# The output product of batch 0 by seven products of halves, with its sums on GpSimd during the mix

## What is computed

```python
def _moe2_ref(x, w_in, w_spatial, b_spatial, w_out):
    h = np.maximum(x @ w_in, 0.0)                   # (2, 768, 1024)
    u, v = h[..., :512], h[..., 512:]
    v_n = (v - mu) / np.sqrt(var + 1e-06)           # over the 512 features
    v_s = np.einsum('ts,bsd->btd', w_spatial, v_n) + b_spatial[None, :, None]   # "the mix"
    gated = u * v_s                                 # (2, 768, 512)
    return (gated @ w_out).astype(np.float32)       # "the output product", 768x512 by 512x512 per batch
```

## Time and profile before

| quantity | value |
|---|---|
| median of three runs | 352.87 us |
| the profiled execution, its own time | 352.47 us |
| its span, first to last instruction | 350.7 us |
| PE busy over the span | 98% |
| DVE busy | 80% |
| POOL busy | 38% |
| last matmul starts | 346.19 us |

### The profile page before, as it was taken

The page is one execution under the profiler, slowest core; times in us unless marked ns, Lnnn a source line. Parts: engine busy times, 40 slices in busy tenths (PEclk is TensorE's granted clock), DMA queues, the critical chain, the costliest instruction groups (busy, mean ns, idle before and its releaser), DMA issues.

```text
span 350.7 us, 7675 instructions
## 1 busy us (share of the span) xinstructions
PE 344.1 (98%) x2890; PEld 315.4 (90%) x2891; DVE 282.0 (80%) x643; ACT 205.5 (59%) x502; POOL 132.7 (38%) x195
## 2 busy tenths in 40 slices
PE   8999999999999999999999999999999999999995
PEld 4568988999989999999989999998899999998894
DVE  6995888777877498899769999956975899949953
ACT  4986767777767489796465556444655107307440
POOL 4889898444554101200034000002464670249300
PEclk9999999999999999999999999999999999999999
DMA  7962343343314023210150000004245500031205
GB/s 234 398 241 69 100 116 91 127 129 120 115 46 168 2 74 135 93 62 0 46 196 0 0 3 0 0 2 164 81 143 155 195 1 2 5 115 61 90 32 186
DMA packets 15915, 33.29 MB, mean 95 GB/s; under 512 B 1921, under 2 KB 6529, under 8 KB 15873
## 3 DMA queue, kind: packets, MB, share of 16 engines
q1 hardware_dynamic: 15440, 32.48, 27.4%
q10 hardware_dynamic: 432, 0.26, 0.3%
HBM read 29.59 MB, written 3.15 MB: 93 GB/s over the span
## 4 chain that ended last, share of the span: by engine, by line
PE 85%; DVE 5%; POOL 5%; ACT 2%; issue 1%; DMA 1%; DVEq 0%; ACTq 0%
PE bank L2236 16%; PE bank L2282 15%; PE bank L2280 15%; PE bank L2281 15%; PE bank L2319 6%; PE bank L2215 4%; PE bank L2191 4%; PE bank L2522 3%; PE bank L2440 3%; PE bank L2317 2%; POOL p_sb L897 2%; PE bank L2145 2%; DVE p_sb L1522 2%; ACT p_sb L1056 1%; PE bank L2521 1%
## 5 line engine op out<-in xcount | busy, mean ns | idle before, releaser
L2236 PE MATMUL bank<-xT,w_hi 128*128 128x384 f32 x256 | 69.6, 345 | 0.2 <-DVE xT L1544 0.2
L897 POOL TENSOR_SCALAR p_sb<-p_sb,denom 128x256 f32<-128x256 f32 (+1 forms) x96 | 48.1, 516 | 35.7 <-DVE denom L1533 35.7
L1056 ACT ACTIVATE p_sb<-p_sb,row_min 128x256 f32<-128x256 f32 (+1 forms) x96 | 46.3, 487 | 14.6 <-DVE row_min L1522 14.6
L2236 PEld LDWEIGHTS bank<-xT,w_hi 128*128 128x128 f32 x256 | 45.7, 188 | 0.7 <-DVE xT L1544 0.4
L2236 PE MATMUL bank<-xT,w_lo 128*128 128x384 f32 x128 | 44.0, 344 | 0.0
L918 POOL TENSOR_SCALAR rstd<-mean_var 128x1 f32<-128x1 f32 x12 | 4.5, 379 | 96.8 <-DVE mean_var L1686 96.8
L1563 DVE SCALAR_TENSOR_TENSOR c_sb<-h_sb,conv_sb,c_sb 128x382 f32<-128x382 f32 (+2 forms) x56 | 37.1, 663 | 2.0
L1522 DVE CUSTOM_DVE_ANT_0 p_sb<-bank,table 128x256 f32<-128x256 f32 (+1 forms) x96 | 33.0, 398 | 5.2 <-PE bank L2145 5.1
L2191 PE MATMUL bank<-ident,p_sb 128*128 128x128 f32 x176 | 29.3, 281 | 0.4 <-POOL p_sb L897 0.2
L1064 ACT COPY pt_sb<-bank 128x512 f32<-128x512 f32 (+1 forms) x44 | 23.9, 544 | 8.5 <-PE bank L2191 8.1
L2191 PEld LDWEIGHTS bank<-ident,p_sb 128*128 128x128 f32 x176 | 20.2, 140 | 7.4 <-POOL p_sb L897 4.4
(11 more groups left out here) (265 smaller groups left out, 992.3 us busy)
## 6 DMA issues: line engine op xcount, KB each, us to landing
stage<-in_weights SPq DMA_DIRECT2D x17, 512.0 KB, 3.3
v_sb<-in_v SPq DMA_DIRECT2D x8, 390.0 KB, 3.8
k_sb<-in_k SPq DMA_DIRECT2D x8, 384.0 KB, 4.2
q_sb<-in_q SPq DMA_DIRECT2D x13, 192.0 KB, 2.4
v_sb<-in_v SPq DMA_DIRECT2D x6, 260.0 KB, 4.5
f_s_raw<-in_weights SPq DMA_DIRECT2D x3, 512.0 KB, 6.0
out_dram<-out_sb SPq DMA_DIRECT2D x6, 256.0 KB, 2.0
k_sb<-in_k SPq DMA_DIRECT2D x5, 256.0 KB, 3.3
```

The source lines that it names most:

```text
L897: nc.gpsimd.tensor_scalar(probs_h, probs_h, denom[:, u % SLOTS, h:h + 1], 1.0, ALU.mult, ALU.mult).then_inc(scaled, 1)
L1056: nc.scalar.activation(p_sb[:, u % SLOTS, h, 0:n], p_sb[:, u % SLOTS, h, 0:n], ACT.Exp, bias=row_min[:, u % SLOTS, h:h + 1], scale=-1.0, a ...
L2236: last = nc.tensor.matmul(h_bank(j)[:, 0:C], w, x, start=r == 0, stop=r == F1_GROUP - 1)
```

## The change

Batch 0's output is made like batch 1's, by one function `output(b)` that runs for both. What that needs is put elsewhere:

- POOL makes the four sums S of batch 0's gated values, `sum_o_s(0)`, as soon as batch 0's gated values and the first pass pair of the second mix are there (the fourth once S1T1 is done), ahead of batch 1's product with u.
- POOL makes the four sums T of the output weights too, after the first two of the eight products with u. DVE made them before.
- The order of products is A11B11, S4B22, S2T2, S3T3, S1T1, A22T4, A12B21 in both batches; S4B22 was fifth.
- DVE makes the rests of six (not eight) blocks of batch 0's gated values, and makes them late; it makes four more rests of sums S and fifteen more additions. ACT makes twelve more copies from bank X and four more rounded sums instead of six copies of whole tiles.
- Both batches are stored in quarters of 128 x 256, 23 of them on SP's queue and one on ACT's. Before, batch 0 had six stores of 128 x 512 and batch 1 nine.

```diff
-O_PASSES = tuple((what, i) for what in ("A11B11", "S2T2", "S3T3", "S1T1", "S4B22", "A22T4", "A12B21") for i in range(OH))
+O_PASSES = tuple((what, i) for what in ("A11B11", "S4B22", "S2T2", "S3T3", "S1T1", "A22T4", "A12B21") for i in range(OH))
-O_X_BANKS, O_BANKS = (4, 5, 6), (7, 0, 1, 2, 3)
-O_SUMS = O_SPLITS = (1, 3, 2, 4)
+O_X_BANKS, O_BANKS = (0, 5, 2), (7, 1, 6, 3, 4)
+O_SUMS, O_S_SPLITS, O_T_SPLITS = (1, 3, 2, 4), (4, 2, 3, 1), (2, 3, 1, 4)
-GT_ROUNDED = tuple((0, n) for n in range(2 * KH)) + tuple((1, k) for k in (0, 1, 4, 5, 6, 7))
-GT_RESTS = GT_ROUNDED[:2 * KH] + tuple((1, k) for k in (0, 1, 5, 7, 4, 6))
+GT_ROUNDED = tuple((0, n) for n in (0, 1, 2, 3, 6, 7)) + tuple((1, k) for k in (0, 1, 4, 5, 6, 7))
+GT_RESTS = tuple((0, n) for n in (0, 1, 6, 7, 2, 3)) + tuple((1, k) for k in (0, 1, 5, 7, 4, 6))
...
 @block.sync
-            for name, k, half, n in (("21", 1, 0, 4), ("12", 0, 1, 3), ("11", 0, 0, 1), ("22", 1, 1, 2)):
-                sp.wait_ge(mix_done, passed("A22T4" if n > 2 else "S2T2", IH - 1))
+            sp.wait_ge(mix_done, passed("S1T1", IH - 1))
+            for name, k, half, n in (("12", 0, 1, 3), ("11", 0, 0, 1), ("22", 1, 1, 2), ("21", 1, 0, 4)):
...
 @block.gpsimd
+            def sum_o_s(b):
+                s1, s2, s3, s4 = (o_s_raw_sb[b][n][:] for n in range(1, 5))
+                nc.gpsimd.tensor_tensor(s1, gt_block(b, 1, 0), gt_block(b, 1, 1), ALU.add).then_inc(o_s_raw, 1)
+                pool.wait_ge(o_s_raw, o_sum_no(b, 1))
+                nc.gpsimd.tensor_tensor(s3, gt_block(b, 0, 0), gt_block(b, 1, 0), ALU.subtract).then_inc(o_s_raw, 1)
...
+                nc.gpsimd.tensor_tensor(s2, s1, gt_block(b, 0, 0), ALU.subtract).then_inc(o_s_raw, 1)
...
+                if b == 0:
+                    pool.wait_ge(mix_done, passed("S1T1", IH - 1))
+                nc.gpsimd.tensor_tensor(s4, gt_block(b, 0, 1), s2, ALU.subtract).then_inc(o_s_raw, 1)
...
 @block.scalar
+            for n in O_S_SPLITS:
+                round_o_s(0, n)
+            for k in (0, 1):
+                round_gt(2 * KH + k)
             act_flag = path_flag(act)
-            for k in (0, 1, 4):
-                round_gt(2 * KH + k)
...
+            act.wait_ge(mix_done, passed("S2T2", IH - 1))
+            for n in O_SUMS:
+                round_o_t(n)
+            act.wait_ge(left_mix, 2 * KH + len(READS))
+            copies_of_x(0)
+            for k in (4, 5, 6, 7):
                 round_gt(2 * KH + k)
...
+            for n in O_S_SPLITS:
+                round_o_s(1, n)
+            copies_of_x(1)
...
 @block.tensor
-            for j in range(NT):
-                result(j)
-            second_output()
+            for b in range(B):
+                output(b)
...
+            def output(b):
+                rests = 6 * b
+                pe.wait_ge(gt_lo_in, rests + 2)
...
+                pe.wait_ge(gt_lo_in, rests + 4)
+                pe.wait_ge(o_t_lo_in, O_T_SPLITS.index(4) + 1)
                 for i in range(OH):
-                    wait_turn("V", i)
-                    o_pass("V", i, gated_tile(1, 1), o_t(4))
-                pe.wait_ge(gt_lo_in, 2 * KH + 6)
+                    wait_turn(b, "V", i)
+                    o_pass(b, "V", i, gated_tile(b, 1, 1), o_t(4))
+                pe.wait_ge(gt_lo_in, rests + 6)
                 for i in range(OH):
-                    wait_turn("Y", i)
-                    o_pass("Y", i, gated_tile(0, 1), out_block(1, 0))
+                    wait_turn(b, "Y", i)
+                    o_pass(b, "Y", i, gated_tile(b, 0, 1), out_block(1, 0))
```

More of the change, by code:

```diff
@@ L838, in _ @@
                                  ).then_inc(again_in[name], 16)
[L839 to L852 removed]
+            for b in range(B):
+                for n, (what, added) in enumerate((("c22", "c22"), ("c12", "c12"), ("c21", "c21"), ("c11", "c11"))):
+                    a, c = int(what[1]) - 1, int(what[2]) - 1
+                    for i in range(OH):
+                        if (b, what, i) == (1, "c11", 1):
+                            continue
+                        sp.wait_ge(o_added, o_add_no(b, added, i))
+                        sp.dma_start(out[b, (a * OH + i) * P:(a * OH + i + 1) * P, c * OW:(c + 1) * OW],
+                                     result_part(b, what, i)).then_inc(stored[(OH * n + i) % 2], 16)
             sp.wait_ge(stored[0], RESULTS[0])
@@ L1953, in _ @@
                 mix_block("c22", "X", i, "S3T3", zv_sb[:, 0, i, :], "z")
-            sum_o_t()
-            for n in O_SPLITS:
-                rest_of_o_t(n)
-            for b, n in GT_RESTS[2 * KH:2 * KH + 2]:
-                rest_of_gated(b, n)
-            for n in O_SPLITS:
-                rest_of_o_s(n)
-            for b, n in GT_RESTS[2 * KH + 2:]:
+            rest_of_o_s(0, 3)
+            rest_of_o_t(3)
+            rest_of_o_t(1)
+            rest_of_o_s(0, 1)
+            for i in range(OH):
+                add_o(0, "c12 R", "R", "S4B22", i)
+            rest_of_o_t(4)
+            for b, n in GT_RESTS[2:4]:
                 rest_of_gated(b, n)
             for i in range(OH):
-                add_o("c22", "Z", "S1T1", i)
-                add_o("c12", "Z", "S1T1", i)
+                add_o(0, "c22", "Z", "S1T1", i)
+                add_o(0, "c12", "Z", "S1T1", i)
+                if i < 2:
+                    rest_of_gated(*GT_RESTS[4 + i])
+            for b, n in GT_RESTS[6:8]:
+                rest_of_gated(b, n)
             for i in range(OH):
-                add_o("c12 R", "R", "S4B22", i)
+                add_o(0, "c21", "V", "A22T4", i)
+            for n in (4, 2):
+                rest_of_o_s(1, n)
             for i in range(OH):
-                add_o("c21", "V", "A22T4", i)
-            for i in range(OH):
-                add_o("c11", "Y", "A12B21", i)
+                add_o(0, "c11", "Y", "A12B21", i)
+            for n in (3, 1):
+                rest_of_o_s(1, n)
+            for b, n in GT_RESTS[8:12]:
+                rest_of_gated(b, n)
+            for i in range(OH):
+                add_o(1, "c12 R", "R", "S4B22", i)
+            for i in range(OH):
+                add_o(1, "c22", "Z", "S1T1", i)
+                add_o(1, "c12", "Z", "S1T1", i)
+            for i in range(OH):
+                add_o(1, "c21", "V", "A22T4", i)
+            for i in range(OH):
+                add_o(1, "c11", "Y", "A12B21", i)
             def general():
```

286 lines of the change are left out of this document (133 added, 153 removed).

## The result

The changed kernel takes 357.43 us (median of 5 runs, 356.54 to 357.76), the kernel before 352.87 us in the same comparison (5 runs, 352.3 to 352.96): a ratio of 1.0132, 95% interval 1.012 to 1.0143, so slower by 4.6 us. The forecast was 358.1 us. The profiled execution took 357.76 us, against the 352.47 us of the one before: +5.29 us. It is the slowest of the five.

The account below looks back on a forecast made before the run. PE was taken as the bound, busy for 98% of the span; -1.85 + 5.4 + 1.1 + 0.5 = +5.2 us on 352.47 us gave 357.7 us, with the median 0.4 us over it 358.1 us; range 354.0 to 361.0 us.

Parts of the forecast that it names:

- The matmuls, -1.85 us: Batch 0's output on PE: at batch 1's price it takes 14.88 us instead of 16.73 us, saving 1.85 us.
- POOL's stream: Added sums S and T (T at 1.7 us each) delay POOL; batch 1's sums start at 323.8 instead of 318.91 us.
- DVE's stream: DVE's rests follow POOL's sums T; bank R additions end at 324.1 us, then three rests take 2.25 us each, to 330.8 us.
- The wait of 5.4 us: PE waits ahead of A22T4 from 325.3 to 330.8 us for DVE's rests beside POOL's sums: 5.4 us.
- 1.1 + 0.5 us of later waits: PE waits 1.1 us ahead of A12B21 for two gated rests and 0.5 us before its third pass for a bank.
- The main case: Whole kernel: matmul saving and PE's waits sum to +5.2 us, giving 358.1 us; chance 50%.
- Rival 3: PE's pause lowers the clock to 1.2 GHz: 2.8 us, partly absorbed by later waits, +1.2 us, 359.3 us; chance 20%.
- The end, 0: After the last matmul, one addition and the last store as before: 0 taken, +0.7 us kept for SP's stores.
- The sum: Whole kernel: -1.85 + 5.4 + 1.1 + 0.5 = +5.2 us on 352.47 us, plus 0.4 us for the median: 358.1 us.
- Rivals 1 and 2: First: turns not lost, 351.0 us, 8%. Second: cheaper POOL sums T and products shorten the wait, 355.1 us, 17%.
- one for one: DVE instructions with both operands in SBUF and POOL instructions take strict turns, each waiting for the other's end.

Follow-up runs that it names:

- experiment 5: Changed kernel with its tail work dealt out anew: GpSimd keeps 8 instructions of 20, DVE does the others in a new order; 351.10 us.
- experiment 4: Kernel before, with only the four sums T moved from DVE to GpSimd, behind its second product with u; 355.02 us.
- Experiment 1: Changed kernel plus 16 matmuls of zeros in batch 0 ahead of A22T4, to fill PE's pause; 356.51 us.
- experiment 6: Changed kernel with the lower half of the output stored in whole rows of 512 columns, 18 stores in place of 24; 357.15 us.
- experiment 2: The held kernel: changed kernel with GpSimd starting batch 1's sums S only after the two gated rests for A22T4 are written; 359.15 us.
- experiment 8: Kernel of experiment 5 with all twenty tail instructions back on GpSimd in the changed kernel's order, DVE's new order kept; 354.94 us.
- experiment 9: Kernel of experiment 5 plus four GpSimd additions of 768 elements that nobody reads; 354.02 us.
- experiment 7: Changed kernel with the two rests of gated values for A22T4 moved ahead of the rest of T2 in DVE's order; 356.30 us.

## Why the prediction was right

- **The matmuls, -1.85 us.** Right; experiment 5 shows them with no wait left: -1.73 us.
- **POOL's stream.** Sums S of batch 0 to 306.1 us (forecast 305.5 to 306); sums T 1.68 us each in the mean (1.7), ended at 315.35 us (315.1); six products 1.34 us each (1.45); batch 1's sums from 323.41 us (323.8). The value chosen between the bounds for the unseen sums T was right to a few hundredths in the mean; the four took 1.29 to 1.89 us. The rows alone put it: near DVE's turn, not near the quiet price that experiment 4 shows (1.29 us).
- **DVE's stream.** Ready for bank R at 324.07 us (323.1): the rest of S1 made PE wait 0.41 us, which I had called just in time. The rest of T4 so began 1.0 us late (325.07, not 324.1 us), but then lost less (1.34 us, not 2.25), and the two gated ones took 2.12 us each. That the two errors cancel but for 0.2 us is luck.
- **The wait of 5.4 us.** 4.95 us, the 0.41 us above among them; A22T4 started at 330.61 us (330.8). That the outputs would start 0.31 us later I had not seen.
- **1.1 + 0.5 us of later waits.** The size was right (1.77 us), the form was not, and that the size held is partly luck. (The terms recorded for the first wait add up to 334.3, not 334.0 us, so 1.4 us.) The main case had no fall of the clock; it fell after the pause, A22T4 took 1.63 us longer, and that covered both. Experiment 1 shows the two as alternatives: at full clock waits of 0.84 and 0.24 us are there, and the total is the same. Rival 3 named this exchange, but had 1.2 us left over; it was 0.0 us in the changed kernel's profiled execution and 1.1 us in that of experiment 6. Its row of slow first matmuls doesn't show the lower clock, though: for 1.3 to 4.0 us of the kernel before the profile gives a granted clock of 1.00.
- **The end, 0.** Right: from the start of the last matmul to the end of the span 356.0 - 351.40 = 4.6 us, 4.5 before, and experiment 6 tells no difference.
- **The sum.** +5.2 us forecast, +5.29 us measured on the profiled execution. I had put the median 0.4 us over the profiled execution, as in the kernel before; it came out 0.3 us under it. That is the 0.7 us between 358.1 and 357.43 us. The changed kernel's executions spread over 1.2 us, those of the kernel before over 0.7 us.
- **Rivals 1 and 2.** The turns were lost; the six products were a little cheaper than taken, too little for 355 us.

The weighing of the Trainium skill, "SBUF — State Buffer", section "SBUF: two separate sides", stands: whoever starts first has the shared pair for the whole instruction. Experiments 2 and 8 agree (0.5 against 2.1 us, 0.95 against 1.76 to 2.59 us). It promises no alternation, and experiment 9, with 5.1 us for one sum, shows that there need be none; my "one for one" went further than the page.

Left open: why DVE kept its turn six times in experiment 9 and lost it mostly in experiment 8, what would come of the new places in the old order, and what sets the length of the low clock (3.4 us in the changed kernel and 6.4 us in experiment 6, behind much the same pause).

## What to carry to other kernels

Before work is moved from DVE to GpSimd, look at DVE's busy share in that stretch and at what it reads: if it is full of instructions with both operands in SBUF, each one handed over can cost DVE more than doing it (here a product with u 0.59 us against up to 1.34 us, a sum of 768 elements 0.95 us against up to 1.85 us). Give GpSimd the few that fall where DVE reads PSUM or stands idle, and put first on DVE what the next product wants. When a wait is taken away, write down which instruction GpSimd or DVE meets next; experiment 2 took away 3.9 us and paid 5.

## What was not expected of the hardware

- The clock: PE stood for 4.1 us until 330.61 us, and only just after it had begun again did the matmuls stand 0.21 us apart in place of 0.118 (18 in 3.76 us), until 334.37 us. In the held kernel PE went on at full pace behind a pause of 2.1 us (it started again at 330.81 us), and slowly behind the next one of 3.0 us (mean granted clock 0.72 in 330 to 335 us and 0.59 in 335 to 340). In experiment 7 matmuls stood 0.21 us apart already behind a pause of 1.8 us, from 332.05 to 335.57 us. So the length of the last pause alone doesn't tell.
- Which of DVE and POOL was first at 275 us, by 0.03 us in one execution and by 0.27 us the other way in another, left both 1.6 us apart at 315 us and until PE's A22T4 at 330 us, in the same code.
